# Attention and two feed-forward layers on one core: the weight splits of the expert stage stand behind the copies of rows on ScalarE and VectorE

## What is computed

```
logits = x @ w_gate                          # x: 1536 x 384
expert_idx = np.argmax(logits, axis=1)
gate_w = probs[np.arange(N), expert_idx]     # softmax of the logits
for i in range(N):                           # tokens in order
    e = expert_idx[i]
    if counts[e] < capacity:                 # capacity 384
        disp[e, counts[e]] = x[i]
        ...
h = np.maximum(np.einsum('ecd,edf->ecf', disp, w1), 0.0)   # w1: 8 x 384 x 1024
y = np.einsum('ecf,efd->ecd', h, w2)                       # w2: 8 x 1024 x 384
out[i] = gate_w[i] * y[expert_idx[i], pos[i]]
```

## Time and profile before

| | us |
|---|---|
| median of 3 runs (525.45 to 529.25) | 528.68 |
| profiled execution, its own time | 528.8 |
| its span, first to last instruction | 527.0 |
| of it from the expert stage's first matmul (at 373.3) on | 153.7 |

### The profile page before, as it was taken

One profiled execution on the slowest core, in us unless ns is written; L12 is line 12 of the kernel. 1 busy time (PEld: TensorE's weight loads), 2 busy tenths in 40 slices (PEclk: granted clock), 3 DMA queues, 4 the chain that ended last, 5 costly groups with the idle time before them and its releaser, 6 DMA issues.

```text
span 527.0 us, 15519 instructions
## 1 busy us (share of the span) xinstructions
PE 473.1 (90%) x6598; PEld 446.0 (85%) x6598; DVE 320.7 (61%) x807; ACT 209.9 (40%) x419; POOL 52.6 (10%) x63
## 2 busy tenths in 40 slices
PE   3779988999999999999999999981899788999994
PEld 3669877999899989998999899981798677989994
DVE  4978974677567756775677546645282676766120
ACT  2422542233323342333243345443355667775220
POOL 5000000000100010001000100202002321132201
PEclk9997988999999999999999999995799988999998
DMA  8745993300040004000000003331647877680000
GB/s 277 281 135 207 320 387 101 137 1 3 33 158 4 1 32 159 3 2 33 3 2 1 33 2 112 103 114 56 236 148 231 269 230 258 211 280 23 25 2 38
DMA packets 34768, 61.33 MB, mean 116 GB/s; under 512 B 3357, under 2 KB 22863, under 8 KB 34689
## 3 DMA queue, kind: packets, MB, share of 16 engines
q1 hardware_dynamic: 32384, 55.71, 31.8%
q0 software_dynamic: 2304, 4.47, 2.3%
HBM read 48.60 MB, written 14.19 MB: 119 GB/s over the span
## 4 chain that ended last, share of the span: by engine, by line
PE 76%; DVE 9%; DMA 5%; issue 5%; ACT 3%; SPq 0%; POOL 0%; ACTq 0%; DVEq 0%; POOLq 0%
PE bank L595 19%; PE bank L583 18%; PE bank L728 7%; PE bank L694 6%; PE pair L493 6%; PE pair L455 3%; DMA stage<-in_moe_w 2%; PE pair L556 2%; DVE W L918 2%; PE pair L551 2%; PE pair L694 2%; PE pair L530 2%; PE pair L728 2%; PE pair L519 1%; PE pair L610 1%
## 5 line engine op out<-in xcount | busy, mean ns | idle before, releaser
L583 PE MATMUL bank<-XH,W 128*128 128x256 f32 x576 | 121.6, 289 | 0.0
L595 PE MATMUL bank<-W,GH 128*128 128x384 f32 x384 | 103.6, 351 | 2.4 <-issue 2.4
L583 PEld LDWEIGHTS bank<-XH,W 128*128 128x128 f32 x576 | 97.9, 195 | 1.0 <-ACT RB L838 0.8
L762 ACT ACTIVATE GH<-GG 128x256 fp32r<-128x256 f32 x96 | 40.1, 418 | 129.3 <-DVE GG L1006 129.3
L583 PE MATMUL bank<-XL,W 128*128 128x256 f32 x288 | 82.3, 286 | 0.0
L1010 DVE TENSOR_TENSOR GL<-GG,GH 128x256 fp32r<-128x256 f32 x96 | 40.7, 424 | 64.2 <-ACT GH L762 64.2
L595 PEld LDWEIGHTS bank<-W,GH 128*128 128x128 f32 x384 | 64.5, 190 | 5.1 <-issue 2.6
L595 PE MATMUL bank<-W,GL 128*128 128x384 f32 x192 | 65.4, 340 | 0.0
L493 PE MATMUL pair<-KRW 48*64 48x32 f32 (+1 forms) x2304 | 46.6, 229 | 11.2 <-DMA KRW<-in_krw 6.7
L583 PEld LDWEIGHTS bank<-XL,W 128*128 128x128 f32 x288 | 56.0, 194 | 0.0
L493 PEld LDWEIGHTS pair<-KRW 48*64 48x64 f32 (+1 forms) x2304 | 41.1, 145 | 17.1 <-issue 6.1
(11 more groups left out here) (153 smaller groups left out, 770.6 us busy)
## 6 DMA issues: line engine op xcount, KB each, us to landing
stage<-in_moe_w SPq DMA_DIRECT2D x32, 768.0 KB
KRW<-in_krw SPq DMA_DIRECT2D x12, 512.0 KB, 5.6
slots<-X SPq DMA_DIRECT2D x1, 4632.0 KB, 19.0
XG<-slots SPq DMA_DIRECT2D x16, 193.0 KB, 2.5
KRW<-in_krw SPq DMA_DIRECT2D x12, 256.0 KB, 5.8
stage<-in_moe_w_in SPq DMA_DIRECT2D x4, 768.0 KB
stage<-in_moe_w_out SPq DMA_DIRECT2D x4, 768.0 KB, 9.2
VV<-in_v SPq DMA_DIRECT2D x12, 240.0 KB, 6.0
```

The costliest lines, as they stand in the source:

```text
L583: last = nc.tensor.matmul(bank[4 + f % 2][:, 0:2 * P], win[wa][:, c, f * P:(f + 1) * P], xa[:, c, :], start=n == 0, stop=n == 3 * KM - 1)
L595: last = nc.tensor.matmul(bank[6 + m][:, 0:DM], ga[f % G4][:, cols], wout[wa][:, f, :], start=f == 0 and n == 0, stop=f == NF - 1 and n == 2)
L762: return nc.scalar.activation(dst, src, ACT.Copy)
```

## The change

On ScalarE and VectorE, the first two splits of each expert's step (chunks 0 and 1 of expert e + 2) leave the hidden part. They stand now behind the copies of the next expert's first two row tiles, chunks 2 and 3 behind the third. ScalarE writes `YO` only for tiles that the expert has; for the others it raises the signal to GpSimd at once, one signal for each tile. On TensorE the first `rows_in` of a small expert moves between the two groups of transposes. SyncE's loads are put in the order in which their buffers come free.

```
@@ SyncE @@
             for e in range(NE):
                 n = CH * (e + 2) + CX
-                load_part(n)
                 load_rows(e + 2, 0)
                 load_rows(e + 2, 1)
+                load_part(n)
                 load_part(n + 1)
+                load_rows(e + 2, 2)
                 load_part(n + 2)
-                load_rows(e + 2, 2)
                 load_part(n + 3)
@@ GpSimd @@
-                    pool.wait_ge(yo_ready, MT * e + m + 1)
+                    pool.wait_ge(yo_ready[m], e + 1)
@@ TensorE, hidden_small @@
                 for c in range(2):
+                    if c == 1:
+                        rows_in(e + 1, 0)
                     pe.wait_ge(rh_ready, 2 * e + c + 1)
@@ ScalarE @@
                     nc.scalar.activation(HH[:, f, :], bank[HB[f % 3]][:, 0:CAP], ACT.Relu).then_inc(hh_ready, 1)
-                    if f in (2, 5):
-                        split_high_expert(e + 2, f // 3)
...
             def hidden_high_small(e):
                 for c in range(2):
-                    split_high_expert(e + 2, c)
...
+            def weighted(e, m):
+                act.wait_ge(y2_done[m], e + 1)
+                act.wait_ge(yo_free[m], e + 1)
+                act.wait_ge(gt_ready, MT * e + m + 1)
+                nc.scalar.activation(YO[m], (bank[6], bank[7], bank[3])[m][:, 0:DM], ACT.Copy,
+                                     scale=GT[e % 2][:, m, 0:1]).then_inc(yo_ready[m], 1)
...
-                for c in range(2, CH):
+                for c in range(2):
                     split_high_expert(e + 2, c)
                 if e + 1 < NE:
                     rows_high(e + 1, MT - 1)
-                for m in range(MT):
-                    act.wait_ge(y2_done[m], e + 1)
...
+                for c in range(2, CH):
+                    split_high_expert(e + 2, c)
+                weighted(e, 0)
+                with act.If(rows > P):
+                    weighted(e, 1)
...
+                with act.Else():
+                    act.sem_inc(yo_ready[1], 1)
+                    act.sem_inc(yo_ready[2], 1)
@@ VectorE @@
-                    if f == 3:
-                        split_low_expert(e + 2, 0)
...
             def hidden_low_small(e):
-                split_low_expert(e + 2, 0)
...
-                split_low_expert(e + 2, 1)
-                split_low_expert(e + 2, 2)
+                for c in range(2):
+                    split_low_expert(e + 2, c)
                 if e + 1 < NE:
                     rows_low(e + 1, MT - 1)
-                split_low_expert(e + 2, 3)
+                for c in range(2, CH):
+                    split_low_expert(e + 2, c)
```

## The result

The changed kernel took 542.32 us in the median (540.31 to 544.74, 4 runs), the kernel before 528.32 beside it (525.45 to 529.25, 4 runs). The ratio is 1.0275 with a 95% interval of 1.0225 to 1.0324: slower by 14 us, where I had forecast 7 and a range up to 542. The profiled execution took 542.49 us with a span of 540.8, and its mean granted clock is 0.946 (before 0.958). A few executions ran slower as a whole (two of e6_second_split_gt3, the profiled one among them, and two of the kernel before on one chip), so the ratios leave them out and no row of e6_second_split_gt3 is used.

A forecast was written before the change was run, and what follows sets the result against it. TensorE was taken to bound the expert stage, except between successive small experts, where ScalarE's split delayed `RH`. Steps summed to +3.6 us and the clock to 3.65, so +7.2 on 528.8: 536, range 530.5 to 542.

The forecast's parts named there:

- The sign: Whole kernel: slower, by 7.2 us; chance of slower 0.59, same 0.34, faster 0.07.
- the scatter's landing: VectorE's `GT` copies wait for the previous expert's scatter, taken as 5 us: 1.7 us more in experts 2 and 3.
- the fourth load: Each small expert's fourth chunk loads only after VectorE's first low split, taking 4.4 us; ScalarE's fourth split waits for it.
- The clock's charge: TensorE at half speed after new idle times: 1.6 us each in experts 4 and 6, 0.45 in expert 3.
- the unblocked chain: From outputs through splits, fourth load and `YO` to the next outputs, without `GT` wait: 13.1 us (small next), 18.2 (two-tile next).
- T: Zero point of the forecast's times: the start of a small expert's outputs on TensorE.
- In expert 5 it costs nothing at 5 us: VectorE's `GT` wait in expert 5: release at T + 16.3 of expert 4, expert 5's outputs at 15.2, cost 0.
- I take 5, in the middle: Scatter's signal 5 us after its start: release at T + 3.2, first low split at T + 3.8 instead of T + 2.1.
- scatters land as slowly as before: Rival: scatter signals take 7.1 us, delaying splits in experts 2, 3 and 5; +13.2 us, 542; chance 0.18.
- I take 4.4: Fourth chunk's load in a small expert's step: issued at T + 3.9, lands 4.4 us later at T + 8.3.
- What costs nothing: Expert 5's step, dropped `YO` copies, moved `rows_in`, SyncE's order and ScalarE's new branches: 0 us.
- the slow-scatter rival: Rival in which scatters take 7.1 us to signal in experts 2, 3 and 5: 542 us, chance 0.18.

The follow-up runs named there:

- e6_second_split_gt3: Kernel before, with ScalarE's second split of a small expert moved behind the row copies and a third `GT` buffer: 525.92 us, ratio 0.9952.
- e1_gt3: Changed kernel with a third `GT` buffer, so the scatter wait reaches one expert further back: 528.4 us, ratio 1.0077 to the kernel before.
- e8_second_split_gt3_yo: Kernel before with ScalarE's second split moved behind the row copies, a third `GT` buffer and `YO` only for existing tiles: 524.44 us, ratio 0.9945.
- e5_yo_before_fourth: Changed kernel with `YO` written ahead of the fourth split, still two `GT` buffers: 532.73 us, ratio 1.009 to the kernel before.

## Why the prediction was wrong

The sign and the mechanism were right, the places nearly so, and the size was half of what came. The steps that failed are two terms of the sum that were too small, the scatter's landing (3.2 us in all) and the fourth load (2.9), and one that was missing, the second tile of expert 4 (0.9). The clock's charge was too small in expert 6 and not felt in expert 3.

**Right: the unblocked chain.** Without the wait at `GT` I had 13.1 and 13.1 us for experts 2 and 3 and 18.2 and 18.2 for 4 and 6; e1_gt3 has 13.25, 13.33, 18.36 and 19.44, the last with 1.2 us of slow clock in it. In the changed kernel expert 2, which no scatter held, has 13.12, and expert 5 has the 15.24 of before. `YO` of expert 1 started at T + 9.7 (row below), forecast T + 9.8:

```profile
415.29 1.49 ACT L764 ACTIVATE WX<-stage 128x1536 fp32r<-128x1536 f32 x1 [1.66 <-DMA stage<-in_moe_w]
416.69 0.56 ACT L893 ACTIVATE x2T<-bank,GT 128x384 f32<-128x384 f32 x1
```

**Wrong: "In expert 5 it costs nothing at 5 us".** I had followed only the first tile of expert 4. It has two, and GpSimd's second scatter began 1.6 us behind the first (a row of its timeline in the changed kernel):

```profile
470.53 1.29 POOL L439 DMA_INDIRECT out<-x2T,GT  x1 [16.25 <-ACT x2T L893]
472.13 0.97 POOL L439 DMA_INDIRECT out<-x2T,GT  x1 [0.30 <-issue]
```

The `GT` copies of expert 5 then waited twice, until 476.76 and 478.65. The first scatter's signal came 6.2 us after its start, the second's 6.5, and each copy waits for its own tile's signal. So the low split was 2.4 us late (T + 4.5 instead of T + 2.1), and with it the fourth load and expert 6. Even scatters of 5 us would have brought the second signal at 477.1, and the undisturbed split would have begun at 474.24 + 2.1 = 476.3, so this step was wrong by its own numbers too, by some 0.9 us. The other 1.5 are the second scatter's 6.5 us instead of 5.

**Wrong: "I take 5, in the middle" for a scatter's landing.** It took 5.8 to 6.5 us. The low split of experts 2 and 3 came at T + 4.7 and T + 4.6 instead of T + 3.8, which is 0.9 and 0.8, and with the 1.5 of expert 5 this is the largest error, 3.2 us. My argument that fewer transfers would be in flight held by half: 7.0 to 7.4 us became 5.8 to 6.5. The rival "scatters land as slowly as before", which gave 542, had the size nearest to the result, but by luck: its 7.1 us were too long, and that made up for the loads and the second tile, which it lacked. The Trainium skill (page "DMA: Bandwidth & Descriptors", section "Anatomy of one DMA — SWDGE (gpsimd) path") would have given 2.45 us, an estimate from its line; the trace contradicts it here with 5.96 and agrees only at the end of the kernel.

**Wrong: "I take 4.4" for the fourth load.** It held in experts 1, 2 and 4 (4.39, 4.59, and 467.70 - 463.07 = 4.63), but took 447.61 - 442.29 = 5.3 in expert 3 and 6.18 in expert 5: +0.9 and +1.8, with the 0.2 of expert 2 together 2.9. In expert 3 a third chunk was issued at 446.16, before this one was in. In expert 5 no other chunk was queued. This table by stretches (busy us of each engine; then granted clock, mean busy share of the 16 DMA engines, GB/s) shows how the load ended:

```profile
482.50:483.50 1.00, 0.40 (x4) 0.19 (x2) 1.00 (x3) 0.00 (x0) 0.00 (x0) 1.00 0.92 313
483.50:484.50 1.00, 0.00 (x0) 0.00 (x0) 0.85 (x1) 0.00 (x0) 0.00 (x0) 1.00 1.00 374
484.50:485.00 0.50, 0.00 (x0) 0.00 (x0) 0.00 (x0) 0.00 (x0) 0.00 (x0) 1.00 0.78 284
485.00:486.00 1.00, 0.00 (x0) 0.00 (x0) 0.00 (x0) 0.00 (x0) 0.00 (x0) 0.84 0.07 28
486.00:486.70 0.70, 0.00 (x0) 0.00 (x0) 0.00 (x0) 0.00 (x0) 0.00 (x0) 0.50 0.07 26
```

From 485 us on the share is 0.07, and one of 16 engines is 0.06: about one DMA engine's worth of work went on for some 1.7 us, while TensorE, VectorE, ScalarE and GpSimd all waited. In it some 46 KB moved (28 GB/s for 1.0 us and 26 for 0.7), nearly the 48 KB that are a sixteenth of the chunk, so by this estimate one engine had most of its part still before it when the others were done. The load of rows issued at 482.71 can have a share in it. The Trainium skill ("DMA: Bandwidth & Descriptors", section "Why a DMA increments its semaphore by 16 and not by 1") says that a transfer counts as landed only once each of its DMA engines has finished; by that rule the load is as long as its slowest engine, and the trace agrees. Why one engine was behind, the trace does not settle.

**Wrong: the clock in expert 6, 1.6 us.** Each idle time was charged 3.2 us at half speed. In expert 6, behind 7.6 us of idle time, it lasted longer. The stretches from the fourth column to the outputs of experts 4 and 6:

```profile
451.40:453.40 2.00, 2.00 (x9) 2.00 (x10) 0.88 (x2) 0.00 (x0) 1.39 (x3) 0.50 0.59 103
453.40:459.00 5.60, 5.60 (x45) 5.60 (x43) 2.23 (x4) 2.34 (x5) 0.88 (x1) 0.86 0.37 135
490.50:494.00 3.50, 3.49 (x16) 3.49 (x17) 1.44 (x3) 0.49 (x1) 2.28 (x3) 0.50 0.06 17
494.00:498.90 4.90, 4.90 (x37) 4.90 (x36) 1.67 (x3) 1.83 (x4) 0.00 (x0) 0.80 0.02 3
```

Expert 4 took 7.6 us for what takes 6.0 undisturbed, so 1.6 as forecast. Expert 6 took 8.4, so 2.4: the granted clock was still 0.50 (1.2 GHz) up to 494.0, and 0.80 in the mean behind it.

**The sum.** Against the forecast's steps (84.9) the measured ones are 7.1 us longer. Expert 3: +0.6 (0.9 for the scatter, 0.2 for its load, less the 0.45 of clock: the slow transposes, 1.05 us at 434.48, were not the ones that the outputs waited for). Expert 4: +1.6 (0.8 for the scatter and 0.9 for the load make 1.7). Expert 6: +4.9 (2.4 for the second tile's signal, 1.8 for the load and 0.8 for the clock make 5.0). The terms add up to 7.3 where 7.1 was measured. "What costs nothing" held for expert 5, which had its 15.24, and for the `YO` and branch edits as far as e8_second_split_gt3_yo shows. In e1_gt3 the charge for the clock shows as a guess: expert 4 paid nothing of its 1.6, expert 6 paid 1.2.

The range ended at the slow-scatter rival's own time, without a bound for the loads. I had seen 6.29 us for a load in the earlier trace rows, if one behind another chunk, and put the term at 4.4 without keeping the longer one as an end: 1.9 us in three steps would have taken the range beyond 545.

## What to carry to other kernels

When a copy or split that frees a buffer moves behind a wait on another engine, follow the new ring once around: here late `YO`, scatter, `GT` wait, late low split, late load, late `YO` again, and each link adds its own delay to the next step. Move only the instruction that stands in the way (here one split of 1.49 us, worth 0.6%), and leave the one that frees the buffer for the next load as early as it was. In such a ring let the longest row seen of each transfer set the end of the range, follow the last tile and not the first, and ask of each wait on a group which member comes last.

## What was unexpected of the hardware

- A 768 KB load took from 4.4 to 6.2 us from issue to use at the same place of the loop, the longest with no other chunk queued and a tail of some 1.7 us at its end, at the busy share of one DMA engine.
- Of the clock: the length of an idle time did not tell its price. In e1_gt3 TensorE idled 2.73 us ahead of the fourth column of expert 4, and the granted clock stayed at 1.00 (2.4 GHz); after 2.65 us of idle time in expert 6 it was 0.56 in the mean. In e5_yo_before_fourth 2.63 us of idle time at the same place were followed by 0.50 (1.2 GHz) from 484 to 488, and the way from the fourth column to the outputs took 8.75 us, 2.7 over the undisturbed 6.0. That is more than the 2.4 behind the 7.62 us of the changed kernel. So for an idle time near 3 us these traces give any price from 0 to 2.7 us. These are the stretches behind the two idle times of e1_gt3, and the row of TensorE in e5_yo_before_fourth:

```profile
445.60:449.00 3.40, 3.37 (x28) 3.37 (x29) 1.87 (x4) 0.98 (x2) 2.31 (x3) 1.00 0.79 239
479.00:482.50 3.50, 3.28 (x17) 3.28 (x18) 1.53 (x4) 0.49 (x1) 2.50 (x3) 0.56 0.06 17
...
483.43 0.58 PE L696 MATMUL bank<-XH,WX 128*128 128x256 f32 x1 [2.63 <-DVE HL L1180]
```
